# An expert's two matrices loaded and counted apart, and the first splits of the last stage's weights moved into and behind the last expert

## The reference

```python
x = attention(q, k, v)            # 8 heads of 64, local window of 96 keys and 8 global ones
e = chosen expert of each token   # argmax of x @ w_gate, or the previous token's
x = p[e] * (relu(x @ w1[e]) @ w2[e])      # w1[e]: 512 x 1024, w2[e]: 1024 x 512, 8 experts
theta = x @ w_theta               # last stage
zr, zi = x * cos(theta), x * sin(theta)
u = x + w_tok_r @ zr + w_tok_i @ zi       # over the 768 tokens of a batch
out = u + relu(u @ w_ch)
```

## Time and profile before

| | us |
|---|---|
| median of 3 runs | 521.57 |
| lowest and highest | 520.28, 522.93 |
| the profiled execution, whole | 522.77 |
| its span in the trace | 519.5 |
| PE busy in it | 494.9 (95%) |
| DVE busy | 271.3 (52%) |
| ACT busy | 198.2 (38%) |
| POOL busy | 104.4 (20%) |

### The profile page before, as it was taken

How to read it: one execution, slowest core, us unless ns; L and a number is a source line. 1 busy time by engine, 2 the same in 40 slices (tenths; PEclk the granted TensorE clock), 3 DMA queues, 4 the chain that set the end, 5 groups by cost and what they waited for, 6 DMA issues and landing times.

```text
span 519.5 us, 9311 instructions
## 1 busy us (share of the span) xinstructions
PE 494.9 (95%) x3356; PEld 431.6 (83%) x3356; DVE 271.3 (52%) x635; ACT 198.2 (38%) x424; POOL 104.4 (20%) x114
## 2 busy tenths in 40 slices
PE   9899999749999999999999889999999999999997
PEld 9678788649999999999899679987888878888885
DVE  4687878774114151414514351468877685445143
ACT  2988887402114141414315231155544332322010
POOL 3998671011111111111111211000000000000000
PEclk9999999959999999999999899999999999999999
DMA  8645318723935556555965401150000000000012
GB/s 336 225 128 199 139 52 314 247 62 124 390 145 210 233 190 250 205 229 209 395 258 189 189 20 40 40 206 1 1 2 0 1 0 21 20 21 20 21 61 81
DMA packets 20696, 71.14 MB, mean 137 GB/s; under 512 B 2734, under 2 KB 5806, under 8 KB 16432
## 3 DMA queue, kind: packets, MB, share of 16 engines
q1 hardware_dynamic: 17872, 63.88, 32.5%
q0 software_dynamic: 2640, 6.30, 3.4%
q10 hardware_dynamic: 144, 0.44, 0.2%
HBM read 62.49 MB, written 10.49 MB: 140 GB/s over the span
## 4 chain that ended last, share of the span: by engine, by line
PE 78%; DVE 10%; ACT 5%; issue 4%; DMA 2%; DVEq 0%; SPq 0%; ACTq 0%
PE ps L1356 43%; PE ps L1385 18%; PE ps L1211 3%; PE ps L1288 3%; PE ps L1251 3%; ACT prob L675 2%; PE ps L1271 2%; DMA w_sb<-in_w_experts 2%; PE ps L1226 2%; DVE w_lo L1091 1%; PE ps L1372 1%; PE ps L1460 1%; PE ps L1421 1%; ACT z_hi L785 1%; DVE z L1133 1%
## 5 line engine op out<-in xcount | busy, mean ns | idle before, releaser
L1385 PEld LDWEIGHTS ps<-xT,w_sb 128*128 128x128 f32 x1024 | 116.6, 192 | 2.5 <-issue 0.8
L1385 PE MATMUL ps<-xT,w_sb 128*128 128x128 f32 x1024 | 117.1, 275 | 0.8 <-DVE xT L1096 0.4
L1082 DVE SCALAR_TENSOR_TENSOR hT_lo<-ps,hT_hi 128x512 fp32r<-128x512 f32 x32 | 21.9, 690 | 97.4 <-ACT hT_hi L729 97.3
L1356 PE MATMUL ps<-w_hi,hT_hi 128*128 128x512 f32 x128 | 51.8, 404 | 4.1 <-DVE hT_lo L1082 4.1
L1091 DVE TENSOR_TENSOR w_lo<-w_sb,w_hi 128x1024 fp32r<-128x1024 f32 x32 | 37.0, 1220 | 27.9 <-ACT w_hi L740 27.9
L675 ACT ACTIVATE prob<-raw,row_min 128x256 f32<-128x256 f32 (+1 forms) x96 | 45.9, 481 | 12.4 <-DVE row_min L927 12.3
L1356 PE MATMUL ps<-w_lo,hT_hi 128*128 128x512 f32 x128 | 50.6, 395 | 0.0
L1356 PE MATMUL ps<-w_hi,hT_lo 128*128 128x512 f32 x128 | 50.6, 395 | 0.0
L729 ACT ACTIVATE hT_hi<-ps 128x512 fp32r<-128x512 f32 x32 | 19.1, 598 | 69.4 <-PE ps L1385 69.4
L733 ACT COPY yout<-ps 128x512 f32<-128x512 f32 x16 | 9.4, 587 | 91.0 <-PE ps L1356 91.0
L740 ACT CAST w_hi<-w_sb 128x1024 fp32r<-128x1024 f32 x32 | 31.1, 1045 | 12.6 <-DVE first_tile L1067 12.5
(11 more groups left out here) (177 smaller groups left out, 940.6 us busy)
## 6 DMA issues: line engine op xcount, KB each, us to landing
w_sb<-in_w_experts SPq DMA_DIRECT2D x32, 1024.0 KB
v_sb<-in_vx SPq DMA_DIRECT2D x8, 640.0 KB, 4.1
q_raw<-in_q SPq DMA_DIRECT2D x8, 384.0 KB, 5.7
x_tok<-y_rows SPq DMA_DIRECT2D x12, 256.0 KB, 4.6
out_x<-o_sb SPq DMA_DIRECT2D x12, 256.0 KB, 2.0
k_raw<-in_kx SPq DMA_DIRECT2D x7, 432.0 KB, 4.7
x_rows<-x_tok SPq DMA_DIRECT2D x2, 1152.0 KB, 11.0
wtr<-in_w_tok_rT SPq DMA_DIRECT2D x6, 384.0 KB
```

Of the source, the lines that this page charges most:

```text
L1082: dve.scalar_tensor_tensor(hT_lo[:, part, :], ps[:, 1 + half, :].rearrange("p (c q) -> p c q", c=4), 0.0, hT_hi[:, part, :].bitcast(F32), ...
L1356: last = pe.matmul(bank, a, b, start=(start and j == 0 and m == 0), stop=(stop and j == count - 1 and m == 2))
L1385: last = pe.matmul(ps[:, 1 + half, f * P:(f + 1) * P], w_sb[:, par, c // 2, j:j + P], xT[:, c, :], start=(c == 0), stop=(c == DC - 1))
```

## The change

There are two parts. The first: an expert's `w1` and `w2` pieces get semaphores of their own (`w1_in`, `w2_in`). SP issues the two `w1` pieces when the hidden values of the last tile of expert e are done (`s_m_h1`), and the two `w2` pieces when its y stage is done. PE waits for `w1_in` alone, ACT for `w2_in` alone. The second: `ahead_of_last` is gone. ACT makes the high parts of `wth` and of row blocks 0 and 1 of `wtr` and `wti` in the tiles of the last expert, between the hidden values and the copy of `yout`; since the loop's length is known only at run time, it repeats them in each of these tiles, to the same places. DVE makes the low parts once, behind its last tile, when `s_first_hi` has counted all tiles.

```diff
-        def each_expert(eng, prepare, tile, ahead):
+        def each_expert(eng, prepare, tile, last_tile):
             def two_experts(pair, last):
                 for par in range(2):
-                    if last:
-                        ahead(par)
                     prepare(pair, par)
...
                     with eng.Fori(begin, end) as t:
-                        tile(pair, par, t)
+                        if last and par:
+                            last_tile(pair, par, t)
+                        else:
+                            tile(pair, par, t)
+                return end
...
+            def next_weights(e, par, done):
+
+                sp.wait_ge(s_m_h1, done)
+                expert_weights(e, par, (0, 1), w1_in)
+                sp.wait_ge(s_m_y, done + 1)
+                expert_weights(e, par, (2, 3), w2_in)
...
-                    sp.wait_ge(s_m_y, done + 1)
-                    expert_weights(2 * pair + par + 2, par)
+                    next_weights(2 * pair + par + 2, par, done)
                     mix_weights(bass.ds(2 * pair + par + 1, 1))
...
+            def expert_tile(pair, par, t):
+                hidden(t)
+                act.sem_inc(s_first_hi, 1)
+                output(t)
+
+            def last_expert_tile(pair, par, t):
+
+                hidden(t)
+                act.wait_ge(s_first_hi, t)
+                act.wait_ge(s_wth_in, 16)
+                act.copy(wth_hi[:], wth[:])
+                act.wait_ge(s_wtr_in, 16 * QT)
+                act.copy(wtr_hi[:, 0:2, :], wtr[:, 0:2, :])
+                act.wait_ge(s_wti_in, 16 * QT)
+                act.copy(wti_hi[:, 0:2, :], wti[:, 0:2, :]).then_inc(s_first_hi, 1)
+                output(t)
...
                 for q in range(4):
-                    act.wait_ge(w_in[par], 64 * (pair + 1))
+                    act.wait_ge(w2_in[par], 32 * (pair + 1))
...
-            def ahead_of_last(par):
-                if par == 0:
-                    act.wait_ge(s_wth_in, 16)
-                    act.copy(wth_hi[:], wth[:]).then_inc(s_w_hi, 1)
-                else:
-                    act.wait_ge(s_wtr_in, 16 * QT)
-                    act.wait_ge(s_wti_in, 16 * QT)
-                    weights_high(0)
...
-            def ahead_of_last(par):
-                if par == 0:
-                    dve.wait_ge(s_w_hi, 1)
-                    low(wth_lo[:], wth[:], wth_hi[:]).then_inc(s_w_lo, 1)
-                else:
-                    weights_low(0)
-
-            each_expert(dve, low_weights, expert_tile, ahead_of_last)
+            tiles = each_expert(dve, low_weights, expert_tile, expert_tile)
...
             weigh(0)
             weigh(1)
-            dve.tensor_copy(wtr_hi[:, 1, :], wtr[:, 1, :])
-            dve.tensor_copy(wti_hi[:, 1, :], wti[:, 1, :]).then_inc(s_w1_hi, 1)
-            weights_low(1)
+            dve.wait_ge(s_first_hi, tiles)
+            low(wth_lo[:], wth[:], wth_hi[:]).then_inc(s_w_lo, 1)
+            weights_low(0)
             x_low(0)
             x_low(1)
+            weights_low(1)
...
             def expert_tile(pair, par, t):
-                pe.wait_ge(w_in[par], 64 * (pair + 1))
+                pe.wait_ge(w1_in[par], 32 * (pair + 1))
                 pe.wait_ge(s_m_xt, t + 1)
```

More of the change, by code:

```diff
@@ L273, in program @@
         s_x2_act = sem("x2_act")
-        s_w1_hi = sem("w1_hi")
+        s_first_hi = sem("first_hi")
         s_e_tx = sem("e_tx")
@@ L306, in program @@
         gathered = [ctx.enter_context(nc.semaphore(f"gathered{n}")) for n in range(NT)]
-        w_in = [ctx.enter_context(nc.semaphore(f"w_in{b}")) for b in range(2)]
+        w1_in = [ctx.enter_context(nc.semaphore(f"w1_in{b}")) for b in range(2)]
+        w2_in = [ctx.enter_context(nc.semaphore(f"w2_in{b}")) for b in range(2)]
         ps = ctx.enter_context(nc.psum_tensor("ps", [P, 8, 512], F32))
@@ L429, in program @@
         tiny = ps[:, 7, GROUP * TURNED:GROUP * TURNED + GROUP * B]
-        def each_expert(eng, prepare, tile, ahead):
+        def each_expert(eng, prepare, tile, last_tile):
             def two_experts(pair, last):
                 for par in range(2):
-                    if last:
-                        ahead(par)
                     prepare(pair, par)
                     begin = end if par else eng.value_load(first_tile[0:1, E - 2:E - 1] if last else
-                                                           first_tile[0:1, bass.ds(2 * pair, 1)], min_val=0,
+                                                           first_tile[0:1, bass.ds(2 * pair, 1)], min_val=E - 2 if last else 0,
                                                            max_val=SLOT_TILES - 1)
@@ L445, in two_experts @@
                     with eng.Fori(begin, end) as t:
-                        tile(pair, par, t)
+                        if last and par:
[3 more added lines that the diff above has]
+                return end
             with eng.Fori(0, E // 2 - 1) as pair:
                 two_experts(pair, False)
-            two_experts(E // 2 - 1, True)
+            return two_experts(E // 2 - 1, True)
         def quarter(w, par, q):
@@ L506, in _, with expert_weights @@
                     sp.dma_start(far[:], far_consts).then_inc(s_rest_in, 16)
-            def expert_weights(e, par):
-                for piece in range(4):
+            def expert_weights(e, par, pieces, landed):
+                for piece in pieces:
                     sp.dma_start(w_sb[:, par, piece, :], w_experts[bass.ds(4 * e + piece, 1)].rearrange(
-                        "o p c -> p (o c)")).then_inc(w_in[par], 16)
+                        "o p c -> p (o c)")).then_inc(landed[par], 16)
+            def next_weights(e, par, done):
[3 more added lines that the diff above has]
+                expert_weights(e, par, (2, 3), w2_in)
             sp.wait_ge(s_rest_in, 16)
             sp.wait_ge(s_x_done, 1)
-            expert_weights(0, 0)
+            expert_weights(0, 0, (0, 1), w1_in)
+            expert_weights(0, 0, (2, 3), w2_in)
             for first, last in ((0, H - 2), (H - 2, H)):
@@ L522, in _ @@
             sp.wait_ge(s_m_xin, 32)
-            expert_weights(1, 1)
+            expert_weights(1, 1, (0, 1), w1_in)
+            expert_weights(1, 1, (2, 3), w2_in)
             sp.dma_start(wth[:], w_theta.rearrange("(c p) d -> p c d", p=P)).then_inc(s_wth_in, 16)
@@ L541, in _ @@
                 done = sp.value_load(first_tile[0:1, e + 1:e + 2], min_val=1, max_val=SLOT_TILES)
-                sp.wait_ge(s_m_y, done + 1)
-                expert_weights(e + 2, e % 2)
+                next_weights(e + 2, e % 2, done)
                 if e == E - 4:
@@ L724, in _, with hidden @@
             act.activation(gate_f[:], gate_e[:], ACT.Exp).then_inc(s_g_act, 1)
-            def expert_tile(pair, par, t):
+            def hidden(t):
                 for half, (done, high) in enumerate(((s_m_h0, s_m_r0), (s_m_h1, s_m_r1))):
@@ L730, in expert_tile, with output @@
                                    ps[:, 1 + half, :].rearrange("p (c q) -> p c q", c=4), ACT.Relu).then_inc(high, 1)
+            def output(t):
                 act.wait_ge(s_m_y, t + 2)
@@ L744, in _ @@
             act.sem_inc(s_y_free, 1)
+            each_expert(act, high_weights, expert_tile, last_expert_tile)
             def weights_high(m):
@@ L753, in weights_high @@
                     act.copy(wch_hi[:], wch[:]).then_inc(s_w_hi, 1)
-            def ahead_of_last(par):
-                if par == 0:
-                    act.wait_ge(s_wth_in, 16)
-                    act.copy(wth_hi[:], wth[:]).then_inc(s_w_hi, 1)
-                else:
-                    act.wait_ge(s_wtr_in, 16 * QT)
-                    act.wait_ge(s_wti_in, 16 * QT)
-                    weights_high(0)
-            each_expert(act, high_weights, expert_tile, ahead_of_last)
             def x_high(n):
@@ L1103, in weights_low @@
             def weights_low(m):
-                if m < 2:
-                    dve.wait_ge(s_w_hi, 2) if m == 0 else dve.wait_ge(s_w1_hi, 1)
-                else:
-                    dve.wait_ge(s_w_hi, m + 1)
+                if m > 1:
+                    dve.wait_ge(s_w_hi, m - 1)
                 if m < QT:
```

## The result

The changed kernel took 516.43 us in the median of four runs (515.86 to 517.26), beside 521.67 us of the kernel before (520.28 to 522.93, four runs): a ratio of 0.9909, 95% interval 0.9891 to 0.9928. The forecast was 516.9, the range 515.0 to 519.3. Two later groups, on other chips, gave a smaller gain with the same kernel: 518.34 us (ratio 0.9940, 0.9919 to 0.9961) and 518.48 us (0.9939, 0.9920 to 0.9959).

What follows compares the result with a forecast made beforehand. PE was taken as the bound, so only its waits and slow-clock stretches could be won: 6.86 us gained less 2.2 at theta(0), about 4.7, putting the median at 516.9 us; 8-in-10 range 515.0 to 519.3.

Steps and rivals of the forecast that it cites:

- The gain of 6.86 us: At experts 5 to 7: 6.23 us from splits leaving the way of experts 6 and 7, 0.63 from earlier loads.
- split clock term of 1.68: Expert 6's y stage: 1.68 us lost to PE's clock at 1.2 GHz after a 2.45 us wait, gone with it.
- the wait of expert 5: PE's wait for expert 5's weights: 0.63 us, to vanish with w1 issued earlier.
- The cost at theta(0), 2.2 us: Start of the last stage: DVE's later low parts delay theta(0) by 2.2 us (0.9 to 3.1), passed on whole.
- A saving is the same against either: Whole kernel: the saving applies equally to the profiled 522.77 us and the median 521.57, so the median goes to 516.9.
- The 4.7: Whole kernel: net saving of 4.7 us, the gain of 6.86 less the delay of 2.2.
- the row of the store: Trace row of an earlier `yout` store beside a two-SBUF-operand DVE subtraction: 1.02 us, no longer than elsewhere, so nothing held.
- the whole-instruction lock: Last `yout` store: DVE subtractions with two SBUF inputs lock GpSimd out, holding it up to 2.29 us; forecast sum unchanged.
- the loads do not lead: Rival at experts 5 and 7: separate counting brings nothing, 1.0 us lost, 517.9 us; chance 0.06.
- the fall at `theta(0)`: Rival: PE's 2.2 us wait before theta(0) drops its clock once, costing 1.68 us, 518.6; chance 0.16.
- one of two such waits had kept its clock: Argument against a clock fall at theta(0): expert 7's 1.65 us wait kept the clock, expert 6's 2.45 did not.

Runs made afterwards that it cites:

- r7: Kernel before with 10 products on the empty tile on PE ahead of expert 6's y stage: 519.76 us, ratio 0.9974.
- r5: Kernel before with only the loads changed (w1 and w2 counted apart, w1 issued at the hidden values' end): 520.20 us, ratio 0.9989.
- r6: Changed kernel with one more 1536-column cast on ACT in each tile of the last expert: 518.65 us, ratio 0.9960.
- r4: Changed kernel with the split of wth one expert earlier, at expert 6: 515.04 us, ratio 0.9883.
- r3: The changed kernel itself, unaltered, timed again on another chip: 518.34 us, ratio 0.9940 to the kernel before.
- r2: Changed kernel with w1 and w2 still counted apart but all four pieces issued together behind the y stage: 518.31 us, ratio 0.9939.
- r9: The changed kernel itself, unaltered, timed once more in a later group: 518.48 us, ratio 0.9939 to the kernel before.
- r1: Changed kernel with the loads as before, four pieces issued together behind the y stage on one semaphore: 519.52 us, ratio 0.9979.

## Why the prediction was right

The first and last hidden values in PE's timeline, before and then after:

```profile
121.27 7.41 PE L1385 MATMUL ps<-xT,w_sb 128*128 128x128 f32 x64 [0.43 <-DVE xT L1096]
...
323.88 7.30 PE L1385 MATMUL ps<-xT,w_sb 128*128 128x128 f32 x64
```

```profile
120.59 7.41 PE L1397 MATMUL ps<-xT,w_sb 128*128 128x128 f32 x64 [0.43 <-DVE xT L1116]
...
316.31 7.30 PE L1397 MATMUL ps<-xT,w_sb 128*128 128x128 f32 x64
```

The last store of `yout` on POOL, after:

```profile
330.95 1.04 POOL L640 DMA_INDIRECT y_rows<-yout,rows_out  x1 [9.83 <-ACT yout L745]
```

- **The gain of 6.86 us.** From the first hidden values to the last the traces have 323.88 - 121.27 = 202.61 us before and 316.31 - 120.59 = 195.72 after: 6.89. Its split clock term of 1.68 measured 1.67 (r7), the wait of expert 5 0.63 (r5).
- **The cost at theta(0), 2.2 us.** Measured 2.11, with the cast at 1.47 us as interpolated, and passed on one to one (r6). That this chain of splits is all of it is shown by r4, where the delay is gone.
- **The sum.** 6.89 - 2.11 = 4.78. The profiled span fell by 5.5; the other 0.7 us lie ahead of the change, where the first hidden values start at 120.59 instead of 121.27.
- **Wrong in the sum: the base.** "A saving is the same against either" does not hold for the 1.68 us of clock, since by their spans about half of the executions of the kernel before have no fall at expert 6 (under r3). Like with like, from the first hidden values to the end, the change is worth 396.56 - 393.41 = 3.15 us where neither kernel has its fall, and 398.23 - 395.04 = 3.19 where both have. The 4.7 is the step from an execution with the fall to one without.
- **Nothing held the last store.** It ran from 330.95 to 331.99, beside the end of `wth_lo` (to 331.12) and the whole of `wtr_lo` (331.04 to 331.99). It took 1.04 us, and tile 2's tokens came 335.81 - 329.55 = 6.26 us after the copy of `yout`, against 6.36 before. So the row of the store decided here, not the whole-instruction lock that the prediction cites from the Trainium skill (SBUF — State Buffer, section "SBUF: two separate sides"). The 2.29 us that the prediction put at that lock were too many for this place anyway, since the store begins 0.17 us before `wth_lo` ends.
- **Mis-sized: the loads.** The rival "the loads do not lead" had 1.0 us; it is 2.08, mainly because expert 7's load needs 14.1 us and not 13.2. I had taken the duration of one load for all. The forecast, in which the wait vanishes anyway, didn't rest on it.
- **Mis-weighed: the clock.** I gave the fall at `theta(0)` 0.16 and priced it at 1.68 us, that is 518.6. The price was right (1.64). The chance was too low: by their spans nine of sixteen executions had it, none of the first four and nine of the twelve after them. The forecast of 516.9 describes the kind without it, and medians of 518.3 and 518.5 the rival. That the first median came out within 0.5 us of the forecast was therefore partly luck; the later ones lie 1.4 and 1.6 us above it, though still in the stated range. The argument against it, that one of two such waits had kept its clock, was worth little.

## What to carry to other kernels

A split, a cast or a copy that is moved off one queue lands on another: find the engine with an idle stretch on each side of the producer, as r4 does, and not only a place in which the first engine is free. Let the part of a load that is wanted first count its own semaphore; that is worth more than issuing it earlier. And price a short wait of TensorE at the wait plus, in a part of the executions, a fall of its clock (1.6 us here), in the kernel before as well as in the changed one. Look at several executions for it, and fill such a wait if it can't be removed: eight more products without use, 13 for 5, kept all six executions here free of it.

## What was not expected of the hardware

The granted clock after a wait differs from execution to execution of one program: after a wait of 2.0 us it fell in three of the five profiled executions with that wait (r2, r3 and r9, at 1.60 to 1.64 us each; not in the first profile and r1), and by the spans in nine of sixteen of the changed kernel. After one of 2.45 us it fell in both that were profiled (the kernel before and r5), yet 31 of 57 executions of the kernel before are too short to have had it. After one of 3.39 us it stayed at 2.4 GHz in the profiled execution. What decides between the two is not settled by these runs. A load of the same four pieces took 13.1 us for expert 5 and 14.1 us for expert 7 (r1); why was not tried.
